# GpSimd's order of work in the expert tiles: ids moved one slot sooner, the rows of the second next tile fetched ahead of the scatter, the scatter's landing awaited at the tile's end

## The reference, cut to what matters

```python
def _moe2_ref(x, modality_id, w_gate, modality_bias, w1, w2):   # x: 3072 x 512, 8 experts, hidden 1024
    logits = x @ w_gate + modality_bias[modality_id]
    e_idx = np.argmax(logits, axis=1)
    probs = softmax(logits)
    gate_w = probs[np.arange(N), e_idx]
    out = np.zeros((N, D), dtype=np.float32)
    for e in range(E):
        mask = e_idx == e
        if not mask.any():
            continue
        h = np.maximum(x[mask] @ w1[e], 0.0)
        out[mask] = gate_w[mask, None] * (h @ w2[e])
    return out
```

## Time and profile before

| | us |
|---|---|
| median of 3 runs (lowest, highest) | 1065.03 (1064.93, 1065.76) |
| profiled execution, its own time | 1065.12 |
| its span in the profile | 1063.4 |
| PE busy in the span | 1050.7 |
| DVE, ACT, POOL busy | 676.4, 469.0, 287.0 |

### The profile page before, as it was taken

How to read it: one execution, slowest core, us unless ns; L and a number is a source line. 1 busy time by engine, 2 the same in 40 slices (tenths; PEclk the granted TensorE clock), 3 DMA queues, 4 the chain that set the end, 5 groups by cost and what they waited for, 6 DMA issues and landing times.

```text
span 1063.4 us, 18502 instructions
## 1 busy us (share of the span) xinstructions
PE 1050.7 (99%) x5886; PEld 904.5 (85%) x5887; DVE 676.4 (64%) x1499; ACT 469.0 (44%) x975; POOL 287.0 (27%) x374
## 2 busy tenths in 40 slices
PE   8999999999999999999999999999999999999997
PEld 7999999888888888888888887888989998999996
DVE  7899999766688578758757767976662222522222
ACT  6888888745443343343343335335352222521122
POOL 6888888501000000000000000422332222223222
PEclk9999999999999999999999999999999999999999
DMA  6677688525220020002002001012381111311100
GB/s 199 204 211 214 203 254 262 175 81 159 80 80 1 1 68 12 1 0 80 1 1 80 1 1 40 5 32 90 121 277 48 52 41 40 102 59 51 46 20 22
DMA packets 57358, 90.72 MB, mean 85 GB/s; under 512 B 11470, under 2 KB 40526, under 8 KB 57168
## 3 DMA queue, kind: packets, MB, share of 16 engines
q1 hardware_dynamic: 50816, 75.17, 22.4%
q0 software_dynamic: 6208, 14.40, 4.1%
q10 hardware_dynamic: 272, 0.39, 0.2%
HBM read 70.86 MB, written 21.69 MB: 87 GB/s over the span
## 4 chain that ended last, share of the span: by engine, by line
PE 91%; POOL 3%; issue 2%; DMA 2%; DVE 1%; ACT 0%; POOLq 0%; SPq 0%; DVEq 0%; ACTq 0%
PE twin L1813 25%; PE bank L1863 13%; PE twin L1863 13%; PE twin L1935 12%; PE twin L1950 12%; PE bank L1735 5%; PE bank L1714 2%; PE twin L1702 2%; PE twin L1701 2%; PE bank L1742 2%; DMA raw_k<-k_twice 1%; POOL k_lo L650 1%; PE bank L1901 1%; PE bank L1752 1%; POOL qs L652 1%
## 5 line engine op out<-in xcount | busy, mean ns | idle before, releaser
L721 POOL DMA_INDIRECT list_scratch<-entry,slot_i x24 | 26.9, 1120 | 472.1 <-DVE slot_i L1460 460.9
L1813 PE MATMUL twin<-x_hi,w_hi 128*128 128x512 f32 x380 | 151.1, 398 | 0.0
L1813 PE MATMUL twin<-x_hi,w_lo 128*128 128x512 f32 x380 | 150.4, 396 | 0.0
L1813 PE MATMUL twin<-x_lo,w_hi 128*128 128x512 f32 x380 | 150.4, 396 | 0.0
L1586 DVE SCALAR_TENSOR_TENSOR g_lo<-twin,g_hi 128x256 fp32r<-128x256 f32 x96 | 40.7, 424 | 143.5 <-ACT g_hi L1016 140.2
L980 ACT ACTIVATE turns<-turns 128x512 f32<-128x512 f32 x96 | 60.7, 632 | 132.1 <-DVE turns L1363 130.9
L1345 DVE CUSTOM_DVE_ANT_0 whole<-y_sb,raw 128x512 f32<-128x512 f32 x160 | 109.7, 686 | 1.9
L1935 PE MATMUL twin<-xg_hi,w_hi 128*128 128x256 f32 x384 | 108.5, 283 | 0.5 <-DVE xg_lo L1486 0.5
L1935 PE MATMUL twin<-xg_lo,w_hi 128*128 128x256 f32 x384 | 108.1, 282 | 0.0
L972 ACT ACTIVATE turns<-twin 128x512 f32<-128x512 f32 x95 | 56.4, 594 | 117.2 <-PE twin L1813 117.1
L1935 PE MATMUL twin<-xg_hi,w_lo 128*128 128x256 f32 x384 | 107.2, 279 | 0.0
(11 more groups left out here) (250 smaller groups left out, 2578.8 us busy)
## 6 DMA issues: line engine op xcount, KB each, us to landing
raw<-w_expert SPq DMA_DIRECT2D x24, 512.0 KB, 6.2
raw_q<-q_twice SPq DMA_DIRECT2D x31, 384.0 KB, 3.7
raw<-w_dense SPq DMA_DIRECT2D x16, 512.0 KB, 4.5
raw_k<-k_twice SPq DMA_DIRECT2D x16, 448.0 KB, 3.8
raw_k<-k_twice SPq DMA_DIRECT2D x16, 416.0 KB, 4.7
v_sb<-v_n SPq DMA_DIRECT2D x16, 384.0 KB, 4.2
xT_scratch<-x_stage SPq DMA_DIRECT2D x16, 384.0 KB, 3.9
x_raw<-xT_scratch SPq DMA_DIRECT2D x6, 1024.0 KB, 5.4
```

What stands on the lines that cost most here:

```text
L1813: last = pe.matmul(hidden_bank(c, f)[:, :], a[:, w], b[:, k, :], start=k == 0 and x == 0, stop=k == KD - 1 and x == 2)
```

## The change

`rows_back` no longer calls `use_entries` nor drains; it waits for `now_made`. `next_rows` is split into `prepare_rows` (hold, take) and `fetch_rows` (wait for `xg_turned`, gather, gates, load). The wait for the scatters stands in `free_rows`, behind `rows_back`. With the new numbering, the round that scatters tile t is: `use_entries` for tile t (held to now), `prepare_rows(t + 1)`, `fetch_rows(t + 1)` (which gathers tile t + 2), scatter tile t, wait for its landing and raise `y_out_free`. `use_entries` for tile 0 comes ahead of the loop, that for the last tile behind it, with the last tile's scatter.

```diff
-            def use_entries(t):
-                pool.wait_ge(held_made, 2 * t + 2)
+            def use_entries(n):
+                pool.wait_ge(held_made, 2 * n)
                 pool.sem_inc(carried_pool, 1)
                 pool.tensor_copy(now_ids[:, :], held_ids[:, :]).then_inc(now_made, 1)
                 pool.tensor_copy(now_gates[:, :], held_gates[:, :]).then_inc(now_made, 1)
...
-            def next_rows(t):
+            def prepare_rows(t):
                 hold_entries(t)
                 take_entries(t + 1)
+
+            def fetch_rows(t):
                 pool.wait_ge(xg_turned, 2 * t + 2)
                 pool.wait_ge(gathered, 32 * t + 32)
                 gather(t + 1)
...
-            def rows_back(t):
-                use_entries(t)
-                pool.drain()
+            def free_rows(n):
+                for j in range(2):
+                    pool.wait_ge(scattered[j], 16 * n)
+                    pool.sem_inc(y_out_free[j], 1)
+
+            def rows_back(n):
+                pool.wait_ge(now_made, 2 * n)
                 for j in (1, 0):
-                    pool.wait_ge(ey_scaled[j], t + 2)
+                    pool.wait_ge(ey_scaled[j], n + 1)
                     pool.sem_inc(carried_pool, 1)
                     pool.indirect_dma_start(
...
-            next_rows(0)
+            prepare_rows(0)
+            fetch_rows(0)
             for j in range(2):
                 pool.sem_inc(y_out_free[j], 1)
-            rows_back(0)
+            use_entries(1)
+            prepare_rows(1)
+            fetch_rows(1)
+            rows_back(1)
+            free_rows(1)
             pool.wait_ge(table_made, 1)
             n_tiles = pool.value_load(table[0:1, T_TILES:T_TILES + 1], min_val=N // TT, max_val=MAXT)
-            with pool.Fori(1, n_tiles) as t:
-                next_rows(t)
-                for j in range(2):
-                    pool.wait_ge(scattered[j], 16 * t)
-                    pool.sem_inc(y_out_free[j], 1)
-                rows_back(t)
+            with pool.Fori(1, n_tiles - 1) as t:
+                use_entries(t + 1)
+                prepare_rows(t + 1)
+                fetch_rows(t + 1)
+                rows_back(t + 1)
+                free_rows(t + 1)
+            use_entries(n_tiles)
+            rows_back(n_tiles)
             for j in range(2):
                 pool.wait_ge(scattered[j], 16 * n_tiles)
```

## The result

The changed kernel takes 1071.12 us (median of 6 runs, 1070.75 to 1071.85), the kernel before 1065.02 in the same comparison: a ratio of 1.0057, 95% interval 1.0045 to 1.0070. It is 6.1 us **slower**. The forecast was 1063.6, and its range ended at 1065.2.

What follows compares the result with a forecast made beforehand. PE, busy 1050.7 of 1063.4 us, was taken as the bound, so POOL counts only where PE waits or behind its last product. Sum: 1065.12 - 1.67 (last tile) + 0.15 (tile 1) = 1063.60; range 1062.7 to 1065.2.

Steps and rivals of the forecast that it cites:

- Drains of tiles 0 to 12: POOL's drains in all tiles but the last: removing them gains nothing, as POOL still waits for the tile's scaling.
- until that load has landed: POOL's tile drains: each seems to last until the entries' load issued just ahead has landed, 3.35 us in tile 13.
- Last tile: Kernel's end: tile 13's real scatter starts 0.90 us after ACT's scaling, at 1058.83 instead of 1060.50, minus 1.67 us.
- Its cause: Tile 13: POOL's lateness, about 1.7 us, came from a 3.35 us drain behind the entries' load.
- Steady tiles: Gather some 8 us sooner, scatter 2.2 us later; nothing in PE's way, zero gain, tile stays at 23.3 us.
- Tile 1: Tile 2's gather delays weight piece 0 by 0.6 us against 0.46 slack, stalling PE: plus 0.15 us.
- Rival B: Weights late in tile 1: stall of 1 to 2.75 us, time 1064.5 to 1066.2; chance 0.13.
- Rival A: Kernel's end stays: what the drain waited for still holds POOL to the same moment, time 1065.0; chance 0.13.
- Rival C: Tile 12's scatter landing delays ids; ACT's start missed above 6.9 us, end later above 7.8; e.g. 1066.3; chance 0.05.
- Rival D: More than the end: PE's short waits, 1.9 us in all, shrink too, by half giving 1062.5; chance 0.12.
- The range: Whole kernel's time, 1062.7 to 1065.2 us; slower by over 0.2%, above 1067.1, got 0.06.

Runs made afterwards that it cites:

- f3: Kernel before, its order kept, with only the drain in rows_back replaced by a wait for now_made; 1071.45 us, ratio 1.0063.
- g3: Kernel before, its order kept, with the drain left out in the last tile only; 1063.99 us, ratio 0.9990.
- h1: Kernel before with only an unused 32-byte-per-partition SBUF pad added behind the small tiles; 1051.28 us, ratio 0.9869.
- h2: Changed kernel with POOL's drain put back at the end of free_rows, plus the 32-byte-per-partition pad; 1049.62 us, ratio 0.9856.

## Why the prediction was wrong

**The step that failed** is "Drains of tiles 0 to 12. Nothing". It treated a drain as a pause: it looked at whom the pause held up, found nobody, and booked zero both for keeping it and for taking it away. The drain is work, 0.040 + 0.080 us per DMA since the last one. Removed from 14 tiles, its work is not gone but gathers at the one that is left, at the program's end, with no cover at all. The prediction had no row for what a drain does once its load has landed. The missing term is 8.08 - 0.22 = 7.86 us. With it the sum would have been 1063.6 + 7.9 = 1071.5, beside 1071.12 measured.

Rows of before said so and were not used. The drain of tile 0, in the trace of the kernel before:

```profile
L788 POOLq DRAIN  x1: 3547/3547/3547, 769.7 to 769.7; - x1
```

The load ahead of it had been issued at 769.35 and landed 2.1 us later, at 771.5, but the drain went on to 773.2 (769.7 + 3.5). Only tile 0's had the list's DMAs ahead of it, 33 DMAs in all. The reading "until that load has landed" fitted 13 drains of 14 and should have been tried on this one. And the end of the program held a drain of its own, 0.216 us, in the rows of line 78; a step that takes out 14 instructions should have looked for a fifteenth that takes over.

**Point by point.**

- *Last tile:* right. Second scatter of tile 12 at 1049.8 forecast, 1048.61 measured (an indirect DMA behind the load follows after 0.31 us, not 1.1); ids moved at 1053.2, measured 1052.2; real scatter of tile 13 ready long before ACT. It starts 1.02 us behind ACT, forecast 0.90. The gain up to POOL's last wait is 1.8 us, forecast 1.67 (0.27 of it is PE's whole path, which ran that much earlier in this execution).
- *Its cause:* right in part. The drain there did wait for a landing. That the new order had a share, because it issues the load sooner, was never needed: f3 and g3 have the gain without it.
- *Steady tiles:* right. A tile lasts 23.36 us (796.34 to 819.70 below), beside 23.34 in the earlier trace rows, and PE waits for nothing new in these tiles.
- *Tile 1:* the term of plus 0.15 was too high. From its first matmul to the next tile's first, PE took 23.62 us, before 23.64:

```profile
772.72 4.51 PE twin L1948 x36
...
796.34 4.26 PE twin L1948 x36
819.70 4.26 PE twin L1948 x36
```

  Piece 0 was not delayed at all: ACT took it 2.53 us after the tile's first matmul (775.25), before 2.64 (775.76), and the second `h_lo` was ready 0.57 us ahead of the matmul that wants it (777.90 to 778.47), before 0.46. What came later was the third piece, for which ACT waited 1.91 us in place of 1.07, while its wait for the fourth fell from 1.85 to 0.92. In all, ACT's waits for weights in this tile grew from 3.8 to 4.1 us, and PE felt none of it. So the step that failed in this term is that the gather would hold up piece 0. The growth agrees with the rule of shared DMA engines (the Trainium skill, DMA: Bandwidth & Descriptors, section Issuing engines are not separate DMA queues), but is too small to prove it. Rival B falls.
- *Rival A* (what the drain waited for stays) was nearest in spirit and wrong in place: POOL was not held in the last tile. *Rival C* (the landing takes the drain's place): in tile 0, beside the weight loads, POOL did wait until 786.68 for a scatter issued at 778.78, 7.9 us, more than the 6.9 that C asks for; in tile 12 it was 3.3, with 4.8 us to spare before ACT's start (1052.2 to 1056.97). *Rival D:* nothing of it; the gain was at the end alone.
- *The range:* its upper end was the time of no change, and for a slower kernel it had only 0.06. With an instruction removed whose function had not been established, a rival of its own for "its work turns up elsewhere" was missing.

## What to carry to other kernels

In these kernels a drain on GpSimd pays for the DMAs that it has issued since the last one, so place it where the engine has time to spare, at best once per round with the transfers landed, and never leave a long row of DMAs to the program's own last drain. Before removing an instruction as idle, ask what it does and which later instance of it will do that instead; the instructions that are not counted as busy, behind the last row of the timeline, are part of the time. And look at the start address of PE's operands: here, reserving 32 unused bytes a partition gave ten times what the whole question about POOL was worth.

## What the runs showed of the hardware that was not expected

- A POOL drain takes 0.040 us plus about 0.080 per DMA issued from POOL since the drain before, from 0 to 100 DMAs, for 8 bytes as for 256 KB, with all of them landed; it waits for those in flight besides (2.48 us behind a 2 KB load, 0.458 without), and for POOL's own computing (3.21 us at line 684, behind four subtractions).
- The dense layer's matmuls of 128x512 in fp32r took 393 to 398 ns in the mean with `x_hi` and `g_hi` at byte addresses that leave 32 when divided by 64, and 389 to 391 at ones that leave 0: 14.0 us of the whole time (h1: 1065.24 to 1051.28). All of it is won before tile 1, which begins at 758.68 in h1 and at 773.12 before. The expert tiles did not gain: from one tile's first matmul to the next's, PE took 23.41 to 23.45 us in h2 and 23.34 to 23.36 before.
- A scatter of 256 KB took 3.3 us from its start until POOL went on in a quiet tile (1048.61 to 1051.91), and 7.9 beside the weight loads of tile 1.
